# Routed experts: the first layer as three single-pass products of split parts

## What is computed

```python
x = attn_out.transpose(0, 2, 1, 3).reshape(1536, 512)        # 1536 tokens, 512 wide
# first mixture: E = 8 experts, each takes exactly cap = 192 tokens
logits = x @ w_gate
order = argsort(-logits.flatten())        # best (token, expert) pairs first
# a pair is taken if the token is free and the expert has room
for e in range(8):
    h = maximum(x[assigned == e] @ w1[e], 0)      # 512 -> 1024
    out[assigned == e] = h @ w2[e]                # 1024 -> 512
# second mixture: 4 experts, all tokens, weighted by domain_probs
out = sum(p[:, e] * (maximum(x @ w1[e], 0) @ w2[e]) for e in range(4))
```

## Time and profile before

| | us |
|---|---|
| median of 3 runs | 1039.59 |
| lowest and highest | 1038.33, 1044.61 |
| the profiled execution's own time | 1038.46 |
| its span, first to last instruction | 1036.7 |
| TensorE busy, of the span | 1002.0 (97%) |
| TensorE weight loads busy | 920.8 |
| VectorE busy | 605.8 |
| ScalarE busy | 444.0 |
| POOL busy | 440.9 |

### The profile page before, as it was taken

How to read it: one execution, slowest core, us unless ns; L and a number is a source line. 1 busy time by engine, 2 the same in 40 slices (tenths; PEclk the granted TensorE clock), 3 DMA queues, 4 the chain that set the end, 5 groups by cost and what they waited for, 6 DMA issues and landing times.

```text
span 1036.7 us, 18055 instructions
## 1 busy us (share of the span) xinstructions
PE 1002.0 (97%) x6542; PEld 920.8 (89%) x6542; DVE 605.8 (58%) x1320; ACT 444.0 (43%) x862; POOL 440.9 (43%) x360
## 2 busy tenths in 40 slices
PE   5999999999998999998999999999999999999996
PEld 4889999999987999998998899998899998899995
DVE  4888888888866444444224555544487544455542
ACT  4888888888830111111333233223253323233320
POOL 5042323233101111112575875565557765576542
PEclk9999999999999999999999999999999999999998
DMA  4223232323155967679921221221212421221201
GB/s 113 74 77 85 76 83 80 80 82 78 30 124 116 228 167 153 206 190 239 210 60 63 79 65 62 82 72 51 83 41 82 142 81 43 82 75 50 80 1 62
DMA packets 87745, 99.62 MB, mean 96 GB/s; under 512 B 18560, under 2 KB 57472, under 8 KB 87680
## 3 DMA queue, kind: packets, MB, share of 16 engines
q1 hardware_dynamic: 84976, 92.40, 33.0%
q0 software_dynamic: 2704, 6.33, 2.0%
HBM read 79.81 MB, written 6.32 MB: 83 GB/s over the span
## 4 chain that ended last, share of the span: by engine, by line
PE 92%; DVE 3%; ACT 2%; DMA 1%; POOL 1%; issue 1%; SPq 0%; DVEq 0%; POOLq 0%
PE ps_y L1431 9%; PE ps_y L1432 9%; PE ps_y L1430 9%; PE ps_h L1457 9%; PE ps_y L1472 7%; PE ps_h L1432 6%; PE ps_h L1430 6%; PE ps_h L1431 6%; PE ps_t L1335 6%; PE ps_s L1322 4%; PE ps_s L1323 3%; PE ps_o L1350 3%; PE ps_o L1349 3%; PE ps_m L1296 2%; PE ps_m L1369 2%; PE ps_m L1282 1%
## 5 line engine op out<-in xcount | busy, mean ns | idle before, releaser
L577 POOL TENSOR_TENSOR w_lo<-w_sum,w_hi 128x1792 fp32r<-128x1792 f32 x32 | 129.8, 4078 | 62.4 <-ACT w_hi L795 62.4
L1432 PE MATMUL ps_y<-b_lo,h_hi 128*128 128x512 f32 x384 | 149.7, 390 | 0.0
L1431 PE MATMUL ps_y<-b_hi,h_lo 128*128 128x512 f32 x384 | 149.7, 390 | 0.0
L1430 PE MATMUL ps_y<-b_hi,h_hi 128*128 128x512 f32 x384 | 149.4, 389 | 0.0
L1249 DVE SCALAR_TENSOR_TENSOR Y<-ps_y,mix_n,Y 128x512 f32<-128x512 f32 x84 | 63.0, 750 | 134.9 <-PE ps_y L1432 134.9
L1430 PE MATMUL ps_h<-x_hi,w_hi 128*128 128x384 f32 x384 | 128.6, 335 | 0.0
L1432 PE MATMUL ps_h<-x_lo,w_hi 128*128 128x384 f32 x384 | 128.5, 335 | 0.0
L1431 PE MATMUL ps_h<-x_hi,w_lo 128*128 128x384 f32 x384 | 128.4, 334 | 0.0
L583 POOL TENSOR_TENSOR b_lo<-b_raw,b_hi 128x2048 fp32r<-128x2048 f32 x16 | 74.0, 4626 | 115.2 <-ACT b_hi L802 115.2
L974 DVE TENSOR_TENSOR p_lo<-ps_t,p_hi 128x384 fp32r<-128x384 f32 x192 | 100.0, 548 | 27.9 <-ACT p_hi L725 26.3
L965 DVE TENSOR_REDUCE neg_max<-ps_s 128x1 f32<-128x768 f32 x96 | 91.3, 951 | 17.9 <-PE ps_s L1323 17.9
(11 more groups left out here) (203 smaller groups left out, 2224.8 us busy)
## 6 DMA issues: line engine op xcount, KB each, us to landing
w_sum<-in_moe_w_dram SPq DMA_DIRECT2D x64, 256.0 KB, 3.2
b_raw<-in_moe_w_dram SPq DMA_DIRECT2D x16, 1024.0 KB, 5.2
raw_a<-in_moe_w_dram SPq DMA_DIRECT2D x8, 1024.0 KB, 8.7
raw_b<-in_moe_w_dram SPq DMA_DIRECT2D x8, 1024.0 KB, 13.0
odd_a<-in_moe_w_dram SPq DMA_DIRECT2D x8, 1024.0 KB, 7.5
odd_b<-in_moe_w_dram SPq DMA_DIRECT2D x8, 1024.0 KB, 14.7
khhT<-kqT SPq DMA_DIRECT2D x32, 192.0 KB, 2.8
raw_k<-in_k_dram SPq DMA_DIRECT2D x16, 192.0 KB, 2.4
```

What stands on the lines that cost most here:

```text
L577: g.tensor_tensor(w_lo[t][:], w_sum[t][:, 1:8], w_hi[t][:].bitcast(F32), ALU.subtract).then_inc(wlo_done[t], 1)
L1430: t_.matmul(dst, w_hi, x_hi, start=first, stop=False)
L1431: t_.matmul(dst, w_lo, x_hi, start=False, stop=False)
L1432: return t_.matmul(dst, w_hi, x_lo, start=False, stop=last)
```

## The change

- The first layer's weights are split: ScalarE copies each [128 x 512] piece to fp32r (`a_hi`), VectorE subtracts that from the piece (`a_lo`), 8 pieces per expert. The rows are split in the same way (`xe_hi` by ScalarE, `xe_lo` by VectorE). `hidden_product` calls `three`: three fp32r matmuls instead of one fp32 product.
- `a_hi` and `a_lo` take memory that `w_lo` and `x_lo` use later, so POOL's `w_low(0, ..)` and VectorE's `x_low(0, ..)` wait for the last hidden product (`h_full` 64).
- The pieces are placed by hand: ScalarE does six ahead of the rows' copy, two behind; VectorE does none, two, three, one and one in the five digits of the next phase, `rows_low` in the third digit, and the eighth piece in the fifth.
- TensorE transposes the next expert's rows after step 52 instead of 61.
- The fill counts are new. A full phase has 64 products as before; phase 1 has 19 instead of 13, phase 2 has 66 instead of 80.
- POOL stores, reads back and fetches the mixing weights in three groups (experts 0 to 4, 5, and 6 to 7), each before the next experts' rows.
- SP's load of expert 6's second-layer weights waits for its rows too.
- After the last phase VectorE writes the ids of expert 6 before it takes the slots of expert 7, with four weight pieces in between.

```diff
-    F_FIRST = (0,) * 6 + (3, 1, 3, 1, 5, 0)
-    F_SECOND = (14, 2, 10, 2, 9, 2, 9, 2, 9, 2, 11, 0)
-    F_PHASE = (12, 2, 7, 2, 6, 2, 6, 2, 6, 2, 9, 0)
-    F_TOKENS = [0, 0, 8] + [8] * (E - 4)
+    F_FIRST = (0,) * 6 + (4, 2, 4, 2, 7, 0)
+    F_SECOND = (8, 2, 8, 2, 8, 3, 6, 3, 6, 3, 8, 0)
+    F_PHASE = (6, 2, 8, 2, 8, 3, 6, 3, 6, 3, 8, 0)
+    F_TOKENS = [0, 0] + [9] * (E - 3)
...
-                if n < E - 2:
+                if n < E - 1:
                     sp.wait_ge(gathered, 32 * (n + 1))
...
+            GROUPS = (E - 3, E - 2, E)
...
             pool.wait_ge(x_stored, 16 * B)
-            for n in range(EARLY):
-                expert_rows(n)
-                keep_ids(n)
-            pool.wait_ge(ids_out[0], 16 * EARLY)
-            ids_by_tile(0, 0, T_EARLY)
-            for n in range(EARLY, E):
-                expert_rows(n)
-                keep_ids(n)
-            pool.wait_ge(mix_stored, 16)
-            pool.wait_ge(ids_back[0], 16)
-            for t in range(T_EARLY):
-                mix_rows(t)
-            pool.wait_ge(ids_out[1], 16 * (E - EARLY))
-            ids_by_tile(1, T_EARLY, NT)
-            pool.wait_ge(ids_back[1], 16)
-            for t in range(T_EARLY, NT):
-                mix_rows(t)
+            for i in range(len(GROUPS)):
+                first, last = ((0,) + GROUPS)[i], GROUPS[i]
+                for n in range(first, last):
+                    expert_rows(n)
+                    keep_ids(n)
+                pool.wait_ge(ids_out[i], 16 * (last - first))
+                ids_by_tile(i, first * CAP // P, last * CAP // P)
+                if i == 0:
+                    pool.wait_ge(mix_stored, 16)
+                pool.wait_ge(ids_back[i], 16)
+                for t in range(first * CAP // P, last * CAP // P):
+                    mix_rows(t)
             for t in range(2):
                 w_sums(0, t)
+            pool.wait_ge(h_full, 8 * E)
             for t in range(2):
                 w_low(0, t)
...
             def rows_1(m):
                 act.wait_ge(xt_full, m + 1)
-                s.copy(xe[:].rearrange("p (a c) m -> p a c m", a=2), xe_ps).then_inc(xe_done, 1)
+                s.copy(xe_hi[:].rearrange("p (a c) m -> p a c m", a=2), xe_ps).then_inc(xe_high, 1)
+
+            def weight_high(m, k):
+                i, a = k // KD, k % KD
+                if a == 0:
+                    act.wait_ge((a_in, odd_a_in)[m % 2][i], 16 * (m // 2 + 1))
+                    at_least(act, h_full, 8 * (m - 1) + 4 * i + 4)
+                s.copy(a_hi[i][:, a, :], (raw_a, odd_a)[m % 2][i][:, a, :]).then_inc(part_hi, 1)
...
             def results_and_rows(n):
+                for k in range(6):
+                    weight_high(n, k)
                 if n > 0:
                     y_out(n - 1, 0)
                 rows_1(n)
+                for k in range(6, 2 * KD):
+                    weight_high(n, k)
                 if n > 0:
                     y_out(n - 1, 1)
...
+            def weight_low(m, k):
+
+                i, a = k // KD, k % KD
+                dve.wait_ge(part_hi, 2 * KD * m + k + 1)
+                v_.tensor_tensor(a_lo[i][:, a, :], (raw_a, odd_a)[m % 2][i][:, a, :], a_hi[i][:, a, :].bitcast(F32),
+                                 ALU.subtract).then_inc(part_lo, 1)
+
+            def rows_low(m):
+
+                dve.wait_ge(xe_high, m + 1)
+                v_.tensor_tensor(xe_lo[:].rearrange("p (a c) m -> p a c m", a=2), xe_ps,
+                                 xe_hi[:].rearrange("p (a c) m -> p a c m", a=2).bitcast(F32),
+                                 ALU.subtract).then_inc(xe_done, 1)
+
+            PIECES = ((), (0, 1), (2, 3, 4), (5,), (6,))
...
+                    if n > 0:
+                        for k in PIECES[i]:
+                            weight_low(n - 1, k)
                     dve.wait_ge(cnt_full, ND * n + i + 1)
                     if i < ND - 1:
...
+                        if n > 0 and i == 2:
+                            rows_low(n - 1)
                         dve.wait_ge(digit_full, ND * n + i + 1)
...
+                        if n > 0:
+                            weight_low(n - 1, 2 * KD - 1)
                         dve.wait_ge(digit_full, ND * n + i + 1)
...
+            token_ids(E - 2)
+            for k in range(KD):
+                weight_low(E - 2, k)
             take_slots(E - 1)
-            token_ids(E - 2)
             slots_hot(E - 1)
             token_ids(E - 1)
+            rows_low(E - 2)
+            for k in range(KD, 2 * KD):
+                weight_low(E - 2, k)
...
             first_x_sums()
+            for k in range(2 * KD):
+                weight_low(E - 1, k)
+            rows_low(E - 1)
+            dve.wait_ge(h_full, 8 * E)
             for k in range(7):
                 x_low(0, k)
...
-                    pe.wait_ge((a_in, odd_a_in)[m % 2][i], 16 * (m // 2 + 1))
+                    pe.wait_ge(part_lo, 2 * KD * m + KD * (i + 1))
...
-                mm = t_.matmul(ps_h[:, H_BANK[j % 3], 0:CAP], wt[i][:, a, f * P:(f + 1) * P], xe[:, a, :],
-                               start=(a == 0), stop=(a == KD - 1))
+                fs = slice(f * P, (f + 1) * P)
+                mm = three(ps_h[:, H_BANK[j % 3], 0:CAP], a_hi[i][:, a, fs], a_lo[i][:, a, fs], xe_hi[:, a, :],
+                           xe_lo[:, a, :], a == 0, a == KD - 1)
...
-                    if st == 2 * S_E - 3 and m < E - 1:
+                    if st == 2 * S_E - 12 and m < E - 1:
                         gathered_rows(m + 1)
```

More of the change, by code:

```diff
@@ L159, in clustered_attention_two_moes @@
         w_hi = [sb(f"w_hi{i}", [P, 7, 2, P], F32R) for i in range(2)]
+        x_hi = sb("x_hi", [P, 7, 2, HC], F32R)
+        parts = ExitStack()
+        a_hi = [sb(f"a_hi{i}", [P, KD, FH], F32R, parts) for i in range(2)]
+        a_lo = [sb(f"a_lo{i}", [P, KD, FH], F32R, parts) for i in range(2)]
+        parts.close()
         w_lo = [sb(f"w_lo{i}", [P, 7, 2, P], F32R) for i in range(2)]
-        x_hi = sb("x_hi", [P, 7, 2, HC], F32R)
         x_lo = sb("x_lo", [P, 7, 2, HC], F32R)
@@ L171, in clustered_attention_two_moes @@
         h1 = sb("h1", [P, 2 * KF, CAP], F32)
-        xe = sb("xe", [P, KD, CAP], F32)
+        xe_hi = sb("xe_hi", [P, KD, CAP], F32R)
+        xe_lo = sb("xe_lo", [P, KD, CAP], F32R)
         logit = sb("logit", [P, NT, E], F32)
@@ L281, in clustered_attention_two_moes @@
         gathered = sem("gathered")
-        ids_out = [sem(f"ids_out{i}") for i in range(2)]
-        ids_back = [sem(f"ids_back{i}") for i in range(2)]
+        ids_out = [sem(f"ids_out{i}") for i in range(3)]
+        ids_back = [sem(f"ids_back{i}") for i in range(3)]
         probs_in = sem("probs_in")
@@ L311, in clustered_attention_two_moes @@
         xe_done = sem("xe_done")
+        xe_high = sem("xe_high")
+        part_hi = sem("part_hi")
+        part_lo = sem("part_lo")
         h_full = sem("h_full")
@@ L600, in expert_rows, with group_of @@
                                          ).then_inc(gathered, 16)
+            GROUPS = (E - 3, E - 2, E)
+            def group_of(n):
+                return sum(n >= last for last in GROUPS)
             def keep_ids(n):
@@ L605, in keep_ids @@
                 g.dma_start(ids_dram[first:first + CAP].rearrange("(s p) o -> p (s o)", s=2), ids[0:CAP // 2, n, :],
-                            allow_slow_non_contiguous=True).then_inc(ids_out[n >= EARLY], 16)
+                            allow_slow_non_contiguous=True).then_inc(ids_out[group_of(n)], 16)
             def ids_by_tile(i, first, last):
@@ L617, in mix_rows @@
                                      ).then_inc(mix_in, 16)
-            EARLY = E - 2
-            T_EARLY = EARLY * CAP // P
             pool.wait_ge(x_stored, 16 * B)
-            for n in range(EARLY):
-                expert_rows(n)
-                keep_ids(n)
-            pool.wait_ge(ids_out[0], 16 * EARLY)
-            ids_by_tile(0, 0, T_EARLY)
-            for n in range(EARLY, E):
-                expert_rows(n)
-                keep_ids(n)
-            pool.wait_ge(mix_stored, 16)
-            pool.wait_ge(ids_back[0], 16)
-            for t in range(T_EARLY):
-                mix_rows(t)
-            pool.wait_ge(ids_out[1], 16 * (E - EARLY))
-            ids_by_tile(1, T_EARLY, NT)
-            pool.wait_ge(ids_back[1], 16)
-            for t in range(T_EARLY, NT):
-                mix_rows(t)
+            for i in range(len(GROUPS)):
[10 more added lines that the diff above has]
+                    mix_rows(t)
             for t in range(2):
                 w_sums(0, t)
+            pool.wait_ge(h_full, 8 * E)
             for t in range(2):
@@ L1445, in hidden_product @@
             def hidden_product(m, st):
-                wt = (raw_a, odd_a)[m % 2]
                 j, a = st // KD, st % KD
```

## The result

The changed kernel took 1052.99 us (median of 5 runs, 1050.67 to 1060.95) against 1039.59 before: ratio 1.0124, 95% interval 1.0086 to 1.0162. It is slower by 1.2%; forecast were 1035.5 us and a range of 1023 to 1048.

What follows compares the result with a forecast made beforehand. TensorE's stream was taken as the bound (busy 1002 of 1036.7 us). Terms 2.8 - 2.6 + 0.3 - 4.9 + 1.7 - 1.0 = -3.7 us gave 1034.8 from 1038.46, stated as 1035.5, range 1023 to 1048.

Steps and rivals of the forecast that it cites:

- The products: First layer on TensorE: three matmuls at 112 ns, 336 against 325 ns per product, +2.8 us over 256 products.
- rival 1: First-layer matmuls: streaming sets the pace at 93 ns, 11.5 us saved, 1022.5 us; chance 0.10.
- rival 2: First-layer matmuls: weight load plus 13 ns, 125 ns each, +12.8 us instead of +2.8, 1046 us; chance 0.15.
- rival 4: First-layer matmuls: two cycles per column, 519 ns per product, +50 us, about 1083 us; chance 0.06.
- 19.8 us better: First-layer products by the skill's gap rule: 82.5 ns per matmul, 248 per product, the sum 19.8 us better.
- Parts inside the phases: Weight copies on ScalarE and subtractions on VectorE during searches: VectorE 12.35 to 19 us per phase, all covered, cost 0.
- Rival 3: Searches: VectorE's chain becomes the bound, phases 2 to 6 each lose 1.5 us, 1043 us; chance 0.12.
- The start: Phases 1 and 2: `slot_ranks` about 1.3 us later, expert 1's rows 0.6 late, net -1.0 us (-2 to +1.5).
- POOL's queue: Mixing rows ahead of expert 5's gather: 2.2 us late against 1.9 spare, +0.3 (0 to 3); next group just fits.
- The last rows: Experts 6 and 7: row wait and half clock gone, -4.9 us; expert 7's slots +1.7; SP's later loads 0, bound +3.
- covered: ScalarE's weight copies waiting for first-layer weights: landed 5 to 9 us after issue, first piece wanted 9 us after `slot_ranks`.
- The second MoE: Start of the second MoE: `w_low` and `x_low` wait for the last hidden product, covered by 10.4 us of output products, 0.

Runs made afterwards that it cites:

- c2: a2 with SyncE's condition and GpSimd's queue exactly as in the kernel before; 1040.66 us, ratio 0.9996.
- e2: c2 without any parts: single fp32 first-layer products, keeping the new distribution, transposes at step 52, last slots and filled waits; 1032.46 us, ratio 0.9916.
- a2: The changed kernel with dummy products filling TensorE's four short waits of phase 1; 1047.18 us, ratio 1.0057.
- a0_again: The changed kernel timed once more, unedited; 1056.88 us, ratio 1.0165.
- e4: e2 with GpSimd's new order of ids and mixing rows and nothing else; 1041.13 us, ratio 0.9995.
- b4: a2 with SyncE's loads for expert 6 no longer held until its rows have come, as in the kernel before; 1041.65 us, ratio 0.9995.
- c3: c2 with expert 7's first layer in fp32 with the rows' high part, and no parts of its weights made; 1036.43 us, ratio 0.9955.
- a3: The changed kernel with every expert's first layer in fp32 with the rows' high part, all parts still made; 1047.4 us, ratio 1.0069.
- a1: The changed kernel with only expert 0's first layer in fp32 with the rows' high part, all parts still made; 1049.84 us, ratio 1.0084.
- d2: The kernel before with GpSimd's new order of ids and mixing rows alone; 1047.2 us, ratio 1.0046.
- e3: e2 with GpSimd's sums for the second MoE ahead of its wait for the last ids; 1033.2 us, ratio 0.9922.

## Why the prediction was wrong

**The products: right.** 112 ns were forecast, a median of 111 measured, so rival 1 (93) and rival 2 (125) are out, and rival 4 too. By the marks an undisturbed expert takes 25.63 us with three matmuls (c2) and 25.39 with fp32 products (e2): 0.24 by 8 is +1.9 us, +2.8 was forecast. The distance is about that of the 32-column matmuls, 112 ns, at six times the columns, so it isn't the streaming that sets it; each of these matmuls has its own weight load, which points to the loads. The Trainium skill ("TensorE: Matmul & The Clock Gate", Back-to-back issue gap) gives the formula behind the prediction's 82.5 ns for the isolated gap, and says itself that at small sizes it comes out too low, because it has no weight load in it; the prediction left that out, and the 111 ns agree with it. Its "19.8 us better" is also the gain over fp32 products: against a sum that holds +2.8 it is 22.6, as its 1014 then has it.

**Parts inside the phases: right.** In experts 1 to 3 VectorE is busy for 18.1 us and ScalarE for 8.7 per expert (54.24 and 26.24 by three; against 12.35 and 4.3), and TensorE waits for nothing. Rival 3 didn't come.

**The start: the step that failed first.** Forecast: -1.0 (-2 to +1.5); measured: +1.8 us before expert 0 and +6.8 in it, and 1.1% by a2 against a0_again. I counted when each result comes, and saw that the split pieces delay `slot_ranks` by 1.3 us. I didn't ask what four waits of about 1 us would do to the clock, although had shown that each wait of 2.4 to 3.2 us is followed by half clock. And I took 3.3 us for the length of such a stretch; here it was 20.5 and 23.9.

**POOL's queue: the second step that failed, one part mis-sized and one part missing.** Forecast: +0.3 (0 to 3). The order alone costs 0.8% (e2 to e4); expert 4's stretch grows by 9.1 us in the changed kernel and by 5.8 in e4. Expert 5's gather was forecast 2.2 us late; in b4 the ids stood at 447.35 and the gather began at 453.61, 6.3 us later. That is the part the sum could have had: the chain from expert 4's ids (421.67) was put at 28 us, and took 20.8 to the first fetch where 18.9 were forecast, and 10.7 for the seven fetches where 9.1 were. Any lateness in it counts in full, since expert 5's gather stands behind all seven in GpSimd's queue. (The next group, put at 24.5 us, comes to 21.5 by the same terms, or 23.7 with the 2.2 us carried on; that it fits stands.) What the sum could not have had is the stop, and in the changed kernel this was the larger part: the ids themselves came only at 462.58 there, and the gather 0.4 us behind them. TensorE's last token matmul had ended at 457.15 and its last first-layer product at 457.91 when VectorE and ScalarE went on:

```profile
457.31 0.25 DVE L1143 TENSOR_TENSOR cand<-m,pick 128x96 bf16<-128x96 f32 x1
462.39 0.15 DVE L1127 COPY place_lo<-ps_h 96x2 f32<-96x2 f32 x1 [4.82 <-remote]
...
465.27 0.33 ACT L833 ACTIVATE h<-ps_h 128x192 f32<-128x192 f32 x1 [9.01 <-remote]
```

and GpSimd issued mixing rows all through it:

```profile
457.79 0.95 POOL L628 DMA_INDIRECT mix_n<-mix_rows,ids_all  x1 [0.30 <-issue]
...
461.54 0.95 POOL L628 DMA_INDIRECT mix_n<-mix_rows,ids_all  x1 [0.30 <-issue]
463.00 1.42 POOL L606 DMA_INDIRECT rows_in<-x_rows,ids  x1 [0.52 <-issue]
```

**The last rows: gained, and lost again.** The 3.2 us wait for rows is gone (-3.4 at expert 5's stretch), as forecast. `slot_hot` of expert 7 cost 0.7 to 1.6 us, forecast 1.7. But SyncE's gate, booked at 0 with a bound of +3, cost up to 0.6% (a2 to b4, see there): the forecast asked only whether odd_a is in when ScalarE wants it, not whether raw_b is in when expert 6's second layer wants it (2.6 us), and the gate was not needed for expert 6's rows: b4 has no wait for them.

**Expert 7's parts.** In the prediction they were part of "covered". They cost 0.4% (c2 to c3): in ScalarE's order the rows' copy stands behind six copies, the last two of which wait for a late load (4.23 us in c2), and it is this load's landing that decides.

**The second MoE: right**, 495.0 us against 495.1, with `w_low` and `x_low` waiting for the last hidden product.

**The sum.** Forecast was -3.7. By the medians, the new distribution, transposes, slots and filled waits bring -8.9 us (e2; the change has no filled waits), all parts cost about 8 (0.8%, e2 to c2), the gate and the order on GpSimd another 0.6% (c2 to a2), and the clock at the start 1.1% (a2 to a0_again). These steps lead from e2 to a0_again's 1.0165, so they add up to it whatever their causes. They also carry a piece that none of the edits touches: in attention, near 32 us, ten of the seventeen profiled executions have 3.4 us at half clock, the changed kernel and a0_again 6.8, and the kernel before, a3 and e2 to e4 none. It can account for the 2.7 us which the changed kernel loses before the first search, and up to 1.7 us of e2's -8.9 may come of it (half of 3.4, an estimate). What decides it is open.

**Not settled.** Why TensorE's results reach VectorE and ScalarE late while GpSimd issues its fetches: VectorE idles for 2.0 to 4.8 us and ScalarE for 3.8 to 9.0 before they go on (changed kernel, a0_again, a2, a3, e4; in a1 only ScalarE, 4.0). It takes no parts (e4), and in the changed kernel it is no instruction load (none from 450 to 479 us takes over 1.3 us). Nor do the fetches always bring it: b4 and d2 have the same seven in the middle of expert 4 and only late rows, and the kernel before, c2 and e2 have nine in a row beside expert 6 without it. But e3, with the same nine, has ScalarE idle for 3.06 us at the ninth. So it is tied to a row of fetches and to something that changes between kernels or executions, which no run here isolates.

## What to carry to other kernels

Moving a block of fetches forward in an in-order queue is priced by what stands behind it: count the whole block against the next item's slack, and look in the other engines' orders for what waits on that queue in turn. A short wait of TensorE is worth its length only if the clock stays: four waits of about a microsecond cost 0.7 to 1.1% here, and filling them with dummy products won it back. And when an edit bundles a new algorithm with a better schedule, run the schedule alone: here it was worth 0.8% (with the filled waits), and the three products with their parts took it all.

## What the runs showed of the hardware

- fp32r matmuls of 192 columns, each with its own weight load of 128 columns, start 109 to 115 ns apart at full clock (median 111), 213 to 214 at half (changed kernel).
- Waits of about 1 us in the same place left the clock at full (a1) or halved it (changed kernel, a0_again, a3). It was back at full after 6.8 us with fp32 products behind the waits (a3), and after 20.5 and 23.9 us with three fp32r matmuls per product behind them.
- With GpSimd issuing indirect fetches back to back, VectorE went on 2.0 to 4.8 us and ScalarE up to 9.0 us after its last work, waiting for results of TensorE that were ready (e4, the changed kernel); in b4 and d2 the same fetches did nothing of the kind.
